# Second unit's dots in front of head 0, and a Fourier stage with its first normalisation split over two engines

## The reference, cut to what matters

```python
q_assign = np.argmax(np.einsum('bhsd,hcd->bhsc', q_n, c_n), axis=-1)
mask = q_assign[:, :, :, None] == k_assign[:, :, None, :]
scores = np.where(mask, scale * np.matmul(q, k.transpose(0, 1, 3, 2)), -1000000000.0)
attn = softmax(scores); out = np.matmul(attn, v)
```

```python
mixed = np.real(np.fft.fft(np.fft.fft(x, axis=1), axis=2))
u = x + mixed
un = (u - mu) / np.sqrt(var + 1e-06)
x = u + np.maximum(un @ w_ch1, 0.0) @ w_ch2
h = np.maximum(x @ w_in, 0.0); out = (h * sigmoid(conv3(h))) @ w_out
```

## Time and profile before

| | us |
|---|---|
| median of 3 runs (687.22 to 689.47) | 688.76 |
| the profiled execution | 687.45 |
| its span | 685.6 |
| TensorE busy | 674.9 |
| VectorE busy | 341.6 |
| ScalarE busy | 276.2 |
| GpSimd busy | 232.7 |

### The profile page before, as it was taken

One profiled execution on the slowest core, in us unless ns is written; L12 is line 12 of the kernel. 1 busy time (PEld: TensorE's weight loads), 2 busy tenths in 40 slices (PEclk: granted clock), 3 DMA queues, 4 the chain that ended last, 5 costly groups with the idle time before them and its releaser, 6 DMA issues.

```text
span 685.6 us, 9772 instructions
## 1 busy us (share of the span) xinstructions
PE 674.9 (98%) x3666; PEld 549.2 (80%) x3666; DVE 341.6 (50%) x662; ACT 276.2 (40%) x586; POOL 232.7 (34%) x253
## 2 busy tenths in 40 slices
PE   7899999999999999999999999999999999999998
PEld 6677776767676789888888888888888899988886
DVE  4887786877876649633113111141111489944300
ACT  5767676767767613111111111121111387734411
POOL 5745878658595050887200000000150070000000
PEclk8999999999999999999999999999999999999999
DMA  5563544425444101344000000010230620000111
GB/s 172 146 151 83 137 141 108 118 65 149 118 128 111 58 1 32 96 119 108 16 1 1 0 1 0 1 62 0 76 109 1 185 62 0 1 32 15 47 47 46
DMA packets 26494, 47.04 MB, mean 69 GB/s; under 512 B 3792, under 2 KB 10832, under 8 KB 26448
## 3 DMA queue, kind: packets, MB, share of 16 engines
q1 hardware_dynamic: 23392, 38.08, 19.9%
q0 software_dynamic: 2912, 7.95, 3.7%
q10 hardware_dynamic: 144, 0.39, 0.2%
HBM read 35.98 MB, written 3.15 MB: 57 GB/s over the span
## 4 chain that ended last, share of the span: by engine, by line
PE 95%; DVE 4%; ACT 0%; issue 0%; POOL 0%; DVEq 0%; POOLq 0%
PE ps L1616 19%; PE ps L1582 19%; PE ps L1664 10%; PE ps L1678 10%; PE ps L1375 10%; PE ps L1361 9%; PE ps L1345 6%; PE ps L1346 5%; PE ps L1462 2%; PE ps L1297 1%; PE ps L1390 1%; PE ps L1517 1%; PE ps L1432 1%; PE ps L1601 1%; PE ps L1314 1%
## 5 line engine op out<-in xcount | busy, mean ns | idle before, releaser
L1175 DVE SCALAR_TENSOR_TENSOR hid_l<-ps,hid_h 128x512 fp32r<-128x512 f32 x48 | 33.2, 691 | 196.6 <-ACT hid_h L819 196.6
L819 ACT ACTIVATE hid_h<-ps 128x512 fp32r<-128x512 f32 x48 | 28.7, 598 | 223.7 <-PE ps L1582 223.7
L1361 PE MATMUL ps<-cst,prob 128*128 128x128 f32 x576 | 81.3, 274 | 0.9 <-DVE pt L945 0.9
L1345 PE MATMUL ps<-k,q 80*128 80x384 f32 x192 | 75.5, 393 | 1.1 <-ACT prob L706 0.8
L1616 PE MATMUL ps<-w_h,hid_h 128*128 128x512 f32 x192 | 76.2, 397 | 0.0
L1616 PE MATMUL ps<-w_h,hid_l 128*128 128x512 f32 x192 | 75.5, 393 | 0.0
L1616 PE MATMUL ps<-w_l,hid_h 128*128 128x512 f32 x192 | 74.7, 389 | 0.0
L1361 PEld LDWEIGHTS ps<-cst,prob 128*128 128x128 f32 x576 | 67.4, 141 | 8.8 <-issue 1.8
L1375 PE MATMUL ps<-pt,v_n 128*64 128x384 f32 x384 | 68.8, 494 | 0.0
L1346 PE MATMUL ps<-k,q 128*128 128x384 f32 x192 | 66.1, 344 | 0.0
L937 DVE TENSOR_REDUCE row_min<-ps 128x1 f32<-128x768 f32 x64 | 61.0, 954 | 7.8 <-PE ps L1346 6.8
(11 more groups left out here) (181 smaller groups left out, 1451.0 us busy)
## 6 DMA issues: line engine op xcount, KB each, us to landing
w_raw<-in_moe_w_ch SPq DMA_DIRECT2D x24, 256.0 KB, 2.6
raw_d<-in_q SPq DMA_DIRECT2D x8, 384.0 KB, 3.4
v_n<-in_v SPq DMA_DIRECT2D x16, 192.0 KB, 2.5
out<-out_s SPq DMA_DIRECT2D x12, 256.0 KB, 2.0
raw_qk<-in_k SPq DMA_DIRECT2D x15, 192.0 KB, 3.2
raw_qk<-in_q SPq DMA_DIRECT2D x15, 192.0 KB, 3.6
q<-q SPq DMA_DIRECT2D x15, 192.0 KB, 3.2
k<-k SPq DMA_DIRECT2D x15, 192.0 KB, 3.7
```

The costliest lines, as they stand in the source:

```text
L1345: nc.tensor.matmul(bank, q2[s][0:D + C, cols], k2[s][0:D + C, keys], start=True, stop=False)
L1361: last = nc.tensor.transpose(ps[:, 4 + hf, j * P:(j + 1) * P], prob[t % 2][:, R * hf + j, :], ident)
```

## The change

The second unit gets raw buffers of its own (raw_e), loaded right behind unit 0's, and bank 6 for its dots. Its dots come before the scores of head 0, its largest dot and hits between the first minima, `first_hit(1)` ahead of VectorE's `step(0, 0, 0)`, and its mask transpose ahead of TensorE's `step(0, 0, 2)`. Unit 0's mask keeps two halves for its largest dots and hits, and does the rest at full width. Filler products are 9 and 2 in place of 4 and 3. In the Fourier stage GpSimd takes two of the four normalisations of the first block, VectorE the other two. The swap of batch 1 goes ahead of them, and the low parts come ahead of the statistics that they stood between.

```diff
+NORM_SPLIT = 2
...
+        raw_e = [sb(pre, f"raw_e{j}", [S]) for j in range(2)]
...
+        def unit_dots(u):
+
+            return ps[:, 6 if u == 1 else 7, 0:4 * NT * C]
...
@@ -445,6 +451,8 @@
 
             sp.dma_start(raw_d[0][:, :], pair_of(q_t, 0)).then_inc(raw_d_loaded[0], 16)
             sp.wait_ge(raw_d_loaded[1], 16)
+            for j, t in enumerate((q_t, k_t)):
+                sp.dma_start(raw_e[j][:, :], pair_of(t, 1)).then_inc(raw_e_loaded[j], 16)
             load_v(0, 0)
             load_k(0, 1)
             sp.dma_start(taps[:, :, :], conv_w).then_inc(taps_loaded, 16)
@@ -453,7 +461,6 @@
             load_q(0, 1)
             sp.wait_ge(k1_first, 1)
             sp.wait_ge(k_split, 1)
-            load_dots(1)
             sp.dma_start(stage[:, 0, 0], w1[0, :, :]).then_inc(w1_raw_loaded[0], 16)
             load_v(0, 1)
             serve(0, 1)
...
+            pool.wait_ge(norm_ready, 1)
+            pool.wait_ge(w1_low, W1_AHEAD + W1_EARLY)
+            for j in range(NORM_SPLIT):
+                nc.gpsimd.tensor_scalar(un[:, j, :], x[:, 0, j, :], ln[:, j, 6:7], ln[:, j, 10:11], ALU.subtract,
+                                        ALU.mult).then_inc(un_ready, 1)
+
             pool.wait_ge(mix_ready, B * UNITS)
...
-                nc.scalar.activation(hit_w[:, :, :].rearrange("p n c -> p (n c)"), ps[:, 7, 0:HALF],
+                nc.scalar.activation(hit_w[:, :, :].rearrange("p n c -> p (n c)"), unit_dots(u),
...
             place_q_rows(0)
+            store_dots(1)
             store_mask(0)
             exponent(0, 0, 0)
-            store_dots(1)
             for t in range(3):
                 step(0, 0, t)
             place_q_rows(1)
...
-            def first_masks(j):
+            def first_hits(j):
 
...
-                dve.wait_ge((half_hit, hit_done)[j], 1)
-                nc.vector.tensor_tensor(hit_w[:, part, :], hit[:, part, :],
-                                        first.unsqueeze(1).broadcast_to([P, 2 * NT, C]),
-                                        ALU.mult).then_inc((half_weighed, hit_w_done)[j], 1)
-                dve.wait_ge((half_weighed, hit_w_done)[j], 1)
-                nc.vector.tensor_reduce(hit_max[:, part], hit_w[:, part, :], axis=AX.X,
-                                        op=ALU.max).then_inc((half_first, hit_max_done)[j], 1)
-                dve.wait_ge((half_first, hit_max_done)[j], 1)
-                nc.vector.tensor_tensor(
-                    mask_n[:, :, j, :, :], first.unsqueeze(1).unsqueeze(1).broadcast_to([P, R, 4, C]),
-                    hit_max[:, part].rearrange("p (a m) -> p a m", a=R).unsqueeze(3).broadcast_to([P, R, 4, C]),
-                    (ALU.is_equal, ALU.not_equal)[j]).then_inc(mask_ready, 1)
...
-                    top = hit_max[:, :].rearrange("p (a j m) -> p a j m", a=R, j=2)[:, :, j, :]
+                    if u:
+                        top = hit_max[:, :].rearrange("p (a j m) -> p a j m", a=R, j=2)[:, :, j, :]
+                    else:
+                        top = hit_max[:, :].rearrange("p (j a m) -> p j a m", a=R, j=2)[:, j, :, :]
                     nc.vector.tensor_tensor(
                         mask_n[:, :, j, :, :], first.unsqueeze(1).unsqueeze(1).broadcast_to([P, R, 4, C]),
                         top.unsqueeze(3).broadcast_to([P, R, 4, C]), op).then_inc(mask_ready, 1)
...
-            first_masks(0)
-            first_masks(1)
+            first_hits(0)
+            first_hits(1)
+            dve.wait_ge(half_hit, 1)
+            weigh_hits(0)
+            first_hit(0)
+            masks(0)
             def place_k_rows(n):
                 dve.wait_ge(mask_turned, n + 1)
                 for tp in range(2):
@@ -1088,14 +1098,14 @@
                                             ALU.mult).then_inc(k_rows_placed, 1)
 
             place_k_rows(0)
-            for t in range(2):
-                minimum(0, 0, t)
+            minimum(0, 0, 0)
+            largest_dot(1)
+            minimum(0, 0, 1)
+            hits(1)
+            first_hit(1)
             step(0, 0, 0)
-            largest_dot(1)
-            hits(1)
+            masks(1)
             step(0, 0, 1)
-            first_hit(1)
-            masks(1)
             step(0, 0, 2)
             place_k_rows(1)
             step(0, 0, 3)
...
+            def swap(b):
+
+                dve.wait_ge(mix_ready, UNITS * b + UNIT_ORDER[b].index(0) + 1)
+                for z in (z_h, z_l):
+                    nc.vector.tensor_copy(z[:, 0:KC + 1, 0], as_f32(z[:, 0:KC + 1, HALF])).then_inc(z_swapped, 1)
...
+                if n == 0 and b == 0:
+                    swap(0)
...
-            def norm(blk):
+            def norm(blk, first=0):
                 if blk:
                     dve.wait_ge(un_turned, KT * blk)
-                for j in range(TBT):
+                else:
+                    dve.wait_ge(norm_ready, 1)
+                    dve.wait_ge(w1_low, W1_AHEAD + W1_EARLY)
+                for j in range(first, TBT):
...
             z_low_part(1, 0)
+            z_low_part(1, 1)
             statistics(0, 0)
-            z_low_part(1, 1)
+            z_low_part(1, 2)
+            z_low_part(1, 3)
             statistics(0, 1)
-            z_low_part(1, 2)
+            z_low_part(1, 4)
             statistics(0, 3)
-            z_low_part(1, 3)
             statistics(0, 4)
             variance(0)
-            z_low_part(1, 4)
             deviation(0)
-            dve.wait_ge(norm_ready, 1)
-            dve.wait_ge(w1_low, W1_AHEAD + W1_EARLY)
-            norm(0)
+            swap(1)
+            norm(0, NORM_SPLIT)
             mix(1, 0)
             mix(1, 3)
             store_un(0)
...
-                pe.wait_ge(mask_stored, u)
-                pe.wait_ge(hit_done, u)
+                if u > 1:
+                    pe.wait_ge(mask_stored, u)
+                    pe.wait_ge(hit_done, u)
                 for j in range(2):
-                    pe.wait_ge(raw_d_loaded[j], 16 * (u + 1))
-                    tiles = raw_d[j][:, :].rearrange("p (a b c) -> p a b c", a=R, b=2)
+                    if u == 1:
+                        pe.wait_ge(raw_e_loaded[j], 16)
+                    else:
+                        pe.wait_ge(raw_d_loaded[j], 16 * u)
+                    tiles = (raw_e if u == 1 else raw_d)[j][:, :].rearrange("p (a b c) -> p a b c", a=R, b=2)
                     for tp in range(2):
                         at = 2 * C * (2 * j + tp)
-                        last = nc.tensor.matmul(ps[at:at + 2 * C, 7, 0:HALF], cen_b[:, u // 2, :], tiles[:, :, tp, :],
+                        last = nc.tensor.matmul(unit_dots(u)[at:at + 2 * C, :], cen_b[:, u // 2, :], tiles[:, :, tp, :],
...
-                    last = nc.tensor.transpose(ps[:, 7, a * P:(a + 1) * P], by_group[:, a * P:(a + 1) * P], ident)
+                    last = nc.tensor.transpose(unit_dots(u)[:, a * P:(a + 1) * P], by_group[:, a * P:(a + 1) * P],
+                                               ident)
...
+                if u == 1:
+                    pe.wait_ge(mask_stored, 1)
...
-            keep_busy(4)
+            keep_busy(9)
             turn_mask(0)
-            keep_busy(3)
+            dots(1)
+            keep_busy(2)
             scores(0, 0, 0)
+            turn_dots(1)
             scores(0, 0, 1)
-            dots(1)
             step(0, 0, 0)
-            turn_dots(1)
             step(0, 0, 1)
+            turn_mask(1)
             step(0, 0, 2)
-            turn_mask(1)
             step(0, 0, 3)
```

More of the change, by code:

```diff
@@ L208, in build @@
         half_dots, half_max, half_hit = sem("half_dots"), sem("half_max"), sem("half_hit")
-        half_weighed, half_first = sem("half_weighed"), sem("half_first")
         q2_first, k1_first, k2_first = sem("q2_first"), sem("k1_first"), sem("k2_first")
@@ L223, in build @@
         raw_d_loaded = [sem(f"raw_d_loaded{j}") for j in range(2)]
+        raw_e_loaded = [sem(f"raw_e_loaded{j}") for j in range(2)]
         q2_masked = [sem(f"q2_masked{s}") for s in range(2)]
@@ L958, in first_masks, with dots_v @@
                                         ALU.is_equal).then_inc((half_hit, hit_done)[j], 1)
-                dve.wait_ge((half_hit, hit_done)[j], 1)
-                nc.vector.tensor_tensor(hit_w[:, part, :], hit[:, part, :],
-                                        first.unsqueeze(1).broadcast_to([P, 2 * NT, C]),
-                                        ALU.mult).then_inc((half_weighed, hit_w_done)[j], 1)
-                dve.wait_ge((half_weighed, hit_w_done)[j], 1)
-                nc.vector.tensor_reduce(hit_max[:, part], hit_w[:, part, :], axis=AX.X,
-                                        op=ALU.max).then_inc((half_first, hit_max_done)[j], 1)
-                dve.wait_ge((half_first, hit_max_done)[j], 1)
-                nc.vector.tensor_tensor(
-                    mask_n[:, :, j, :, :], first.unsqueeze(1).unsqueeze(1).broadcast_to([P, R, 4, C]),
```

(14 more changed lines are left out.)

## The result

The changed kernel takes **695.43 us** (median of four runs, 694.98 to 695.62) against 688.88 us for the kernel before on the same chip (four runs, 687.22 to 689.47). The ratio is 1.0093, with an interval of 1.0071 to 1.0116, so it is 6.5 us slower by the medians. The direction was forecast, the size was not: 691.2 us was the forecast, and the time lies above the range's upper end of 694.0. The profiled execution took 695.62 us with a span of 693.8, against 685.6 before.

The account below looks back on a forecast made before the run. TensorE, busy 674.9 of 685.6 us, was taken as the bound. Losses of 1.05 (opening's wait), 1.2 (clock) and 0.15 us (Fourier stage) sum to 2.4, on 688.76 giving 691.2 us; range 687.7 to 694.0.

Parts of the forecast that it names:

- GpSimd's price: Fourier stage: one normalisation on GpSimd takes 0.6 us, bounded by a two-input instruction's 1.34 us.
- The collision: Fourier stage: VectorE and GpSimd normalisations lock a shared port pair and run one after the other, done at about 270.1.
- The moved swap: Fourier stage: swap moves to about 268.4, mix(1,0) starts at 270.0 against 269.25; the stage loses 0.15 us.
- The opening: Front of the kernel: first_hit(1) waits for GpSimd, scores of head 1 come 1.05 us later, plus 1.2 us for the clock.
- GpSimd on q at 12.8: Opening: q of head 1 lands at 12.8 us behind the two new loads, 0.7 us later; bounds 0 and 1.1.
- TensorE idle some 4 us, clock down near 20 or 21: Opening: TensorE idles ahead of tile 1's right half turn until 22.3 us, and the clock falls near 20 or 21 us.
- The clock's cost of 1.2 us: Opening: slow clock after the new idle delays head 1's scores by 1.2 us; bounds 0 and 4.
- The clock does not fall at 10.8 us: Opening: five more fillers cover 1.4 of the 1.7 us idle, so the early fall of the clock goes.
- A: Opening: the clock stays up through the new idle, 1.2 us lost, 690.0 us; chance 0.15.
- B: Opening: the clock stays low past tile 3 of head 1, 694 us; chance 0.12.
- C: Opening: the two new loads don't delay q of head 1, 690.6 us; chance 0.13.
- D: Opening: hit_w isn't last, VectorE's idle of some 2.7 us is filled, 686.1 us, faster; chance 0.10.

Follow-up runs that it names:

- g4: Changed kernel with GpSimd's two normalisations multiplying twice by one, leaving out the real normalisation of two tiles; 690.34 us in one run.
- e3: Changed kernel with constants as operands of GpSimd's two normalisations, leaving out the real normalisation of two tiles; 693.98 us, 1.0081 of the kernel before.
- e4: Changed kernel with one normalisation on GpSimd and three on VectorE; 691.56 us, 1.0044 of the kernel before.
- f4: Kernel before with only the swap and the low parts moved, all normalisations on VectorE; 688.97 us, 1.0009 of the kernel before.
- e1: Changed kernel with all four normalisations of the first block on VectorE, new opening kept; 691.59 us, 1.0039 of the kernel before.
- f3: e1 with q of head 1 issued right behind the two new loads, ahead of k, v and the taps; 689.10 us, 1.0014 of the kernel before.
- g1: e1 with q of head 1 right behind the two new loads and the second unit's hit_w product on VectorE; 688.63 us, 0.9999 of before.
- g2: g1 with 5 and 0 filler products in place of 9 and 2; 689.57 us, 1.0007 of the kernel before.

## Why the prediction missed

**The step that failed: GpSimd's price.** The prediction took 0.6 us for a normalisation, with 1.34 as its bound; it measured 2.66 and 2.07. The price came from a tensor_scalar of 64x768 and a two-input instruction of 128x512. But every tensor_scalar that GpSimd ran in the kernel before multiplies twice by constants, and none subtracts. g4 shows that for two multiplications the estimate was near (0.79 to 0.92 us). From this one term follow the 2.95 us of added wait and, as the idle of 3.56 us brought the clock down, 1.29 us more: 4.2 us where 0.15 stood, with 0.7 as its worst. In g4, with the cheap pair, the clock stays up, so the second loss hangs on the first; no rival had either. The profiled spans differ by 8.2 us: 3.24 in the opening, 4.24 here, 0.3 for the moved swap, and 0.4 left. Among that are waits for xt_l in the second MLP, 0.9 us against 0.3; they lie between 0.3 and 1.1 us in all profiles here, and their cause was not traced.

**The collision: right that there is one, wrong in who pays.** VectorE's two normalisations were not delayed (0.54 us each). GpSimd's first took 2660 ns and its second, mostly beside VectorE's mix, 2067: 0.59 us more, about one VectorE normalisation. In the earlier trace rows the second of VectorE's two began at 309.88, 0.12 us behind GpSimd's, and took 1.51 us, until 0.29 us after its end; here VectorE's first began 0.14 us ahead. In e3 the price is shared: VectorE's second takes 835 ns, 0.29 more, beside a GpSimd instruction of 2.22 us, and so does its third in e4, beside one of 2.66. The Trainium skill, page "SBUF — State Buffer", section "Who interferes with whom", says that issue order decides who blocks, and that the loser blocks for the whole instruction. The trace agrees with the first for the instruction that VectorE began ahead, but its second began 0.3 us behind GpSimd's and was not delayed either. Against the second speaks e3, where VectorE lost 0.29 us and not the rest of the 2.22. What decides who pays here stays open.

**The moved swap** was costed nearly right (forecast 0.15 us lost): f4's transposes start at 270.29 against 270.46, though its opening ends 0.1 us later, and its first up product at 274.23 against 273.82, as the mix comes later. That is some 0.3 us, too little for its ratio of 1.0009 to show.

**The opening: mechanism right, one term short.** Forecast 2.25 us later for the scores of head 1 (26.75 to 29.0), measured in e1 29.93, that is 3.18. By steps:
- GpSimd on q at 12.8, upper bound 13.2: 14.17 in e1, 13.67 in the kernel after. This is the mis-sized term, by 0.9 to 1.4 us; q came 4.6 to 4.9 us after its issue against 3.1 before. A slip in the sum is 0.3 of it: 140 KB at the rate of 1,216 KB in 6.1 us are 0.7 us and not 0.4. The rest may be that this rate came from a queue with data in flight (DMA share 0.59 at 10 us), where e1 begins with none (0.00 from 6 to 7 us); that was not tested.
- first_hit(1) at 20.3: 21.73, later by what q is later.
- From there to the end of tile 3's minimum 3.7 us: 25.11 + 0.16 - 21.73 = 3.54.
- TensorE idle some 4 us, clock down near 20 or 21: 3.28 us, and down at 23.2.
- The clock's cost of 1.2 us: without it the scores would stand at 25.27 + 3.8 = 29.07, so it was 0.86.
- "The clock does not fall at 10.8 us": wrong. In e1 it was at 1.2 GHz from about 9.2 to 12.6 us, with TensorE busy without a gap since 6.47. That should have cost nothing there, as the hits were done at 18.57 us and GpSimd began its product at 20.71.

In the changed kernel's own profile another link was last, the late hits, and no clock fell behind first_hit(1). It ends within 0.04 us of e1 at the values (35.57 and 35.53). So the opening's 3.2 us can come by either way, and what shortens one alone need not shorten the other.

**The rivals.** A (clock stays up) fell with e1, whose clock falls in the new idle. In the changed kernel's own profile it does stay up, which the prediction named as a sign of being wrong; there the slow dots cost as much. B (clock low past tile 3 of head 1) came nearest in time, 694 us, for the wrong reason: in e1 the clock is back at 29.7 us, ahead of head 1's scores, and the second clock loss lies in the Fourier stage. C (no delay of q) fell with e1, where q comes 2.05 us later than before; f3 takes the delay away and by the ratios some 1.7 us of the time with it. D (the change does what it moves for) fell with e1 too, where VectorE waits for hit_w, and g1 shows that even without this wait nothing is gained.

## What to carry to other kernels

Before work is moved to another engine, look in the trace for that engine running the same operations, not only the same shape: here the same tile cost 0.79 or 1.91 us by the pair of operations alone. Then ask how long the dense engine would stand still if the price were several times the estimate (here 3.4 to 4.4 times), and add the clock if that idle is longer than one that has already brought it down. When a wait is moved ahead of other work on an in-order engine, check each link of the chain that feeds it, the loads that it now queues behind among them.

## What was not expected of the hardware

- GpSimd on a 128x512 float32 tile: subtract then multiply 2.07 us, with constants 1.91, multiply twice 0.79; VectorE does the first in 0.54.
- An idle of 1.48 us in the Fourier stage left the clock up (e4); one of 2.92 us brought it down (e3, 12 transposes in 2.82 us), and so did 3.56. In the opening 1.77 us left it up (g1) and 2.30 brought it down (g2).
- The clock fell at 9.2 us in e1 while TensorE worked without a gap, where the kernel before, idle at 9.4, kept it until 10.8. In g2, with five fillers and an idle of 1.64 us ahead of the first mask's transpose, it reads 1.00 until 21 us. What sets the opening's clock from one execution to the next stays open.
- In the kernel after the granted clock reads 1.00 from 8 to 16 us while 24 dots take 5.33 us, against 2.89 in e1. Durations are the safer witness there.
